# Two small VectorE instructions moved behind the weight sums of the same step

## The reference

```python
attn = chunked linear attention with decay lam per head    # (B, H, S, 64)
x = attn.transpose(0, 2, 1, 3).reshape(B, S, 512)
u = x + real(fft(fft(x, axis=1), axis=2))
mu = mean(u, -1); var = mean((u - mu) ** 2, -1)
un = (u - mu) / sqrt(var + 1e-6)
x = u + maximum(un @ w_ch1, 0) @ w_ch2                     # 512 -> 2048 -> 512
gate = sigmoid(causal conv of x, 5 taps, per channel)
out = (gate * (x @ w_val)) @ w_out
```

## Time and profile before

| | |
|---|---|
| median of 3 runs | 427.87 us (427.77 to 427.97) |
| the profiled execution | 427.97 us, span 426.3 us |
| TensorE busy | 418.8 us, 98% of the span |
| VectorE busy | 281.3 us, 66% |
| ScalarE busy | 187.0 us, 44% |
| GpSimd busy | 211.4 us, 50% |
| granted TensorE clock | 9 (full) in all 40 slices |

### The profile page before, as it was taken

The page is one execution under the profiler, slowest core; times in us unless marked ns, Lnnn a source line. Parts: engine busy times, 40 slices in busy tenths (PEclk is TensorE's granted clock), DMA queues, the critical chain, the costliest instruction groups (busy, mean ns, idle before and its releaser), DMA issues.

```text
span 426.3 us, 6828 instructions
## 1 busy us (share of the span) xinstructions
PE 418.8 (98%) x2626; PEld 353.6 (83%) x2626; DVE 281.3 (66%) x451; ACT 187.0 (44%) x354; POOL 211.4 (50%) x139
## 2 busy tenths in 40 slices
PE   8999999999999999989999999999999999999997
PEld 8788888788888888879898988888788888888886
DVE  5658989759345579948667652617998859669400
ACT  2355842584213457474644432254254342624212
POOL 3543431443876396857787793445645338300000
PEclk9999999999999999999999999999999999999999
DMA  7997801430420231232232323321321321002022
GB/s 235 352 330 228 255 3 33 144 120 8 143 98 24 78 100 49 92 106 99 100 100 98 101 98 110 119 81 64 121 68 37 100 93 49 0 2 99 0 100 98
DMA packets 14863, 44.09 MB, mean 103 GB/s; under 512 B 1904, under 2 KB 2160, under 8 KB 14832
## 3 DMA queue, kind: packets, MB, share of 16 engines
q1 hardware_dynamic: 14832, 43.67, 30.9%
HBM read 40.52 MB, written 3.15 MB: 102 GB/s over the span
## 4 chain that ended last, share of the span: by engine, by line
PE 81%; DVE 12%; ACT 2%; DMA 2%; issue 2%; SPq 1%; DVEq 0%; ACTq 0%
PE ps L732 8%; PE ps L734 8%; PE ps L733 8%; PE ps L661 6%; PE ps L669 6%; PE ps L662 6%; PE ps L568 3%; PE ps L840 3%; PE ps L839 3%; PE ps L838 3%; PE ps L816 3%; PE ps L530 3%; PE ps L817 3%; PE ps L818 3%; PE ps L676 3%; PE ps L675 3%
## 5 line engine op out<-in xcount | busy, mean ns | idle before, releaser
L984 ACT ACTIVATE hh<-ps 128x512 fp32r<-128x512 f32 x32 | 18.9, 603 | 88.3 <-PE ps L669 88.3
L1358 DVE SCALAR_TENSOR_TENSOR hl<-ps,hh 128x512 fp32r<-128x512 f32 x32 | 21.6, 688 | 49.2 <-ACT hh L984 49.2
L1442 DVE SCALAR_TENSOR_TENSOR xT<-u_pad,cw,xT 128x768 f32<-128x768 f32 (+2 forms) x48 | 52.6, 1164 | 0.0
L1595 POOL TENSOR_TENSOR w2l_b<-raw_b,w2h_b 128x1024 fp32r<-128x1024 f32 x12 | 30.7, 2557 | 32.3 <-ACT w2h_b L947 32.3
L1595 POOL TENSOR_TENSOR w2l_a<-raw_a,w2h_a 128x1024 fp32r<-128x1024 f32 x12 | 31.1, 2592 | 29.9 <-ACT w2h_a L947 26.4
L732 PE MATMUL ps<-hh,w2h_a 128*128 128x512 f32 x96 | 37.9, 395 | 1.6 <-DVE xT L1374 1.6
L732 PE MATMUL ps<-hh,w2h_b 128*128 128x512 f32 x96 | 38.1, 397 | 0.1
L734 PE MATMUL ps<-hh,w2l_b 128*128 128x512 f32 x96 | 37.9, 395 | 0.0
L733 PE MATMUL ps<-hl,w2h_b 128*128 128x512 f32 x96 | 37.9, 395 | 0.0
L734 PE MATMUL ps<-hh,w2l_a 128*128 128x512 f32 x96 | 37.5, 391 | 0.0
L733 PE MATMUL ps<-hl,w2h_a 128*128 128x512 f32 x96 | 37.5, 390 | 0.0
(11 more groups left out here) (252 smaller groups left out, 1193.0 us busy)
## 6 DMA issues: line engine op xcount, KB each, us to landing
raw_a<-in_mlp SPq DMA_DIRECT2D x25, 512.0 KB, 3.6
raw_b<-in_mlp SPq DMA_DIRECT2D x23, 512.0 KB, 3.6
chunks<-in_qkv SPq DMA_DIRECT2D x12, 512.0 KB, 6.4
chunks<-in_qkv SPq DMA_DIRECT2D x22, 256.0 KB, 5.7
out<-out_sb SPq DMA_DIRECT2D x11, 256.0 KB, 2.0
raw_a<-in_val SPq DMA_DIRECT2D x2, 512.0 KB, 3.7
raw_b<-in_out SPq DMA_DIRECT2D x2, 512.0 KB, 5.5
seq_c<-const_seq SPq DMA_DIRECT2D x1, 768.0 KB, 7.9
```

The costliest lines, as they stand in the source:

```text
L984: nc.scalar.activation(hh[:, slot, j], ps[j][:, :], ACT.Relu).then_inc(s_hh, 1)
L1358: stt(hl[:, slot, j], ps[j][:, :], 0.0, hh[:, slot, j].bitcast(F32), ALU.max, ALU.subtract).then_inc(s_hl, 1)
L1442: stt(xT[:, b, r, tok], u_pad[b][:, r, PAD - d + tok.start:PAD - d + tok.stop], cw[:, K - 1 - d, r:r + 1], xT[:, b, r, tok], ALU.mult, ALU ...
L1595: tt(lo, raw_, hi.bitcast(F32), ALU.subtract).then_inc(s_w2l, 1)
```

## The change

In VectorE's `mlp_step`, the calls `add_eps(2)` and `add_eps(3)` of step 6 move from a place ahead of `combine_weights(st.m + 3)` to a place behind it (and behind everything else of the step). Nothing else of step 6 stands between the two places, since step 6 is not the last of its token block. The orders of the other engines, and all waits and counts, are the same.

```diff
@@ -1481,9 +1481,6 @@
                     add_eps(0)
                     add_eps(1)
                     tokens_lo()
-                if st.m == 6:
-                    add_eps(2)
-                    add_eps(3)
                 if seven(st.m + 3):
                     combine_weights(st.m + 3)
                 if st.last:
@@ -1515,6 +1512,9 @@
                 if st.m == 5:
                     for part in range(3):
                         newton(0, part)
+                if st.m == 6:
+                    add_eps(2)
+                    add_eps(3)
                 if st.m == 17:
                     x3_lo(0)
                     x3_lo(1)
```

## The result

| | median | range | executions |
|---|---|---|---|
| before | 427.87 us | 427.69 to 428.24 | 5 |
| changed | 430.36 us | 429.87 to 431.29 | 5 |

The ratio is 1.0062, 95% interval 1.0048 to 1.0077: the change costs 2.5 us, where 1.0 us was forecast. The mechanism of the forecast is there at every step; the case that it held for unlikely, a fall of TensorE's clock after the stall, came on top in all 8 executions of the changed kernel whose granted clock is listed. The profiled execution of the changed kernel took 431.07 us (span 429.3), 3.1 us more than that of before; 0.55 us of this is there ahead of the edit already (GpSimd's long instruction, L1595, starts at 176.39 instead of 175.84), so I compare distances and not positions.

The account below looks back on a forecast made before the run. TensorE, busy 98% of the span, was taken to bound the kernel. A 3.69 us lateness less 0.36, 0.46 and 1.86 us gave +1.01, so 428.9 us; own range 428.3 to 429.4, 8 in 10 428.1 to 430.5.

Parts of the forecast that it names:

- Step 1: VectorE's four weight sums, held by GpSimd's instructions, end no earlier: 0 us gained, bounds 0 and 0.93 us.
- Step 2: On VectorE, the two add_eps start behind the fourth sum, take 1.00 us and end at 180.42 instead of 175.60 us.
- Step 3: TensorE's third product group of first_products(8) waits for add_eps; its second product starts 3.69 us late.
- Step 4: Three TensorE waits behind the stall close when TensorE is late, giving back 0.36, 0.46 and 1.86 us.
- the holes: TensorE's waits after 178.17, 186.14 and 189.58 us, for GpSimd, VectorE and scale_finished: 0.36, 0.46 and 1.86 us.
- Step 5: From 191.8 us on nothing is given back; the long VectorE stretch from 291 us moves as a whole.
- The sum: Whole kernel: TensorE's lateness less the three waits, +3.69 - 0.36 - 0.46 - 1.86 = +1.01 us.
- rival (c): TensorE leaves the stall at a slower clock for 3 to 6 us, losing 1.3 to 2.6 us more; 12%.

Follow-up runs that it names:

- e4_short_lo7: The changed kernel with GpSimd's second_lo(7) subtracting only 32 of its 1024 columns: 426.48 us, ratio 0.9968.
- e8_after_one: The kernel before with both add_eps moved behind the first of the four weight sums only: 427.83 us, ratio 1.0004.
- e3: The kernel before with VectorE's newton(0) moved from step 5 to step 7, behind first_sums(8): 426.01 us, ratio 0.9954.
- e1_fill24: The changed kernel with the second product group of step 8 done five times instead of once, 24 more products: 429.15 us, ratio 1.0025.
- e12: The kernel before with ScalarE's inverse_root(1) moved from ahead of seven_hi(8) to behind first_hi(10), in step 7: 425.72 us, ratio 0.9946.
- e15: The changed kernel with ScalarE's inverse_root(1) moved from ahead of seven_hi(8) to behind first_hi(10): 431.35 us, ratio 1.0066.
- e14: The changed kernel with the second product group of step 8 done four times instead of once, 18 more products: 428.83 us, ratio 1.0024.
- e5: The kernel before with both add_eps moved behind the second of the four weight sums only: 429.61 us, ratio 1.0039.
- e10: The changed kernel with newton(0) moved to step 7, and second_hi(7) and second_lo(7) moved from step 6 to step 5: 428.51 us, ratio 1.0009.
- e9: The kernel before with newton(0) moved to step 7, and second_hi(7) and second_lo(7) moved from step 6 to step 5: 426.19 us, ratio 0.9963.

## Why the prediction was wrong

- **Step 1, the sums gain nothing**: right. The fourth sum ends 1.07 us after GpSimd's long instruction (1.08 before), the first grew from 0.64 to 1.56 us. e4_short_lo7 shows that GpSimd's instruction is the cause, e8_after_one that the time of the two add_eps fits into the held time. That the size was right has a condition that the step took as given: nothing moved had been holding GpSimd. Where it is newton(0) that is moved (e3), GpSimd's instruction itself ends earlier.
- **Step 2**: right, 1.01 us behind the fourth sum.
- **Step 3, TensorE 3.69 us late**: right, 3.66 (3.68 in e1_fill24).
- **Step 4, the holes give back 2.68 us**: right. All three are gone in the trace of after, where the slow stretch may have had a part in it, and in that of e1_fill24, where it had none: 2.65 us. e12 with e15 shows that two of them are the same 2.3 us.
- **Step 5**: right. The one later wait, at the long VectorE stretch, is 0.3 us in the kernel before and in every other one here.
- **The sum and the rivals**: wrong, and this is the step that failed. The sum has no term for the products after the restart; it lets them run 0.12 and 0.23 us apart, and they ran 0.21 and 0.43 apart for 3.4 us, which cost 1.5 us. This was rival (c), at 12%, with 430.2 to 431.5 us, and its case came in all 8 executions whose clock is known. The range of 8 in 10, 428.1 to 430.5, holds the measured 430.36 only because it reached into (c); the forecast's own range, 428.3 to 429.4, does not. I let "no row between 10 and 420 us shows such a fall" speak against it. That was no evidence: no row there shows an idle stretch over 1.62 us either, so the trace of before was silent on it, and the rule of the Trainium skill (TensorE: Matmul & The Clock Gate, Part 1) should have weighed more. The size of (c), 1.3 to 2.6 us, was right: 1.5 us in the profiled execution, and about 2.5 between the executions with 0.992 (431.29 to 431.46) and those of full clock (428.8 in e14 and e15). In part this was luck. The slow row that its 43% came from, 5.26 us in the earlier trace rows, has a granted clock of 1.00 in its profile, so it shows no fall, and no row gave the length of 3 to 6 us.
- With the clock kept full the forecast holds: 429.15 against 428.12 us in e1_fill24, 428.83 against 427.84 in e14_fill18. So the missing term is the whole error, to within about 0.1 us.

What stays open is what decides in a given execution whether the clock falls at 2 to 3.4 us of idle time, how long it then stays at half, and why the times at 0.996 are spread (430.03 and 431.31 in e15).

## What to carry to other kernels

When an edit makes TensorE stand, price two things: the lateness, less the holes behind that a late TensorE closes, and the half clock afterwards. The second does not show in a trace that has no idle stretch of that length; do not read its absence as safety. And an instruction that looks slow beside another engine's may be waiting for it: moving work into that held time is free (e8_after_one), and taking other work away from in front of it gains nothing as long as the instruction that holds it ends when it did (the change). It gains where the work taken away had been holding that instruction (e3_before_newton7, 1.9 us).

## What the runs showed of the hardware

- The clock falls late: 0.9 us after the restart in the profiled execution of after, about 0.4 us after it in that of e5 (its third product, at 180.09, already takes 0.36 us instead of 0.28), and in the last part of the idle time in that of e15. So most of the price is paid on useful products, and it differs between executions of one kernel.
- 2.00 us of idle time was enough in 5 of 6 executions, 1.62 us in none of 57.
- Twelve useless products in a hole of 3.4 us saved the clock in 1 of 6 executions, eighteen and twenty-four in all: 430.43, 428.83 and 429.15 us.
- GpSimd and VectorE hold each other both ways: a sum takes 2.62 us instead of 0.42, and GpSimd's 128x256 subtraction 1.46 instead of 0.75. In the rows of before and after, one VectorE instruction with two SBUF inputs passes between two of GpSimd's. The last instruction of newton(0) takes 0.96 us in e10, where GpSimd is idle, 1.39 in the kernel before and 2.49 in e3 and e9, beside GpSimd's.
